# Fourier matmuls placed between the heads of a recurrence kernel's chunk loop, and small zero products in batch 0

## What is computed

```python
# B, H, S, D = 4, 8, 768, 48; DM = H * D = 384
scale = np.minimum(mag, 0.999) / (mag + 1e-06)          # mag = |a|
for t in range(S):                                       # complex decay per key dimension
    new_re = ar * S_re - ai * S_im
    new_im = ar * S_im + ai * S_re
    S_re, S_im = (new_re + kv, new_im)                   # kv = k_t outer v_t
    y[:, :, t] = np.einsum('bhd,bhde->bhe', q[:, :, t], S_re)
x = y as (B, S, DM)
u = x + real(fft(fft(x, axis=1), axis=2))                # Fourier mixing
u = u + relu(layernorm(u) @ w_ch1) @ w_ch2               # 384 -> 1536 -> 384
h = relu(u.T @ w_tok1) @ w_tok2, u = u + h.T             # second block: token mixing
out = u + relu(u @ w_ch1') @ w_ch2'
```

## Time and profile before

| What | Value |
|---|---|
| three timed runs | 1131.98, 1138.62, 1141.57 us; median 1138.62 |
| profiled execution | 1134.15 us, span 1132.4, mean TensorE clock 0.928 of full |
| busy share of the span | PE 89%, PEld 86%, DVE 48%, ACT 30% |
| edited phase | 0 to about 417 us |

### The profile page before, as it was taken

How to read it: one execution, slowest core, us unless ns; L and a number is a source line. 1 busy time by engine, 2 the same in 40 slices (tenths; PEclk the granted TensorE clock), 3 DMA queues, 4 the chain that set the end, 5 groups by cost and what they waited for, 6 DMA issues and landing times. The chain is left out here.

```text
span 1132.4 us, 15567 instructions
## 1 busy us (share of the span) xinstructions
PE 1008.8 (89%) x6082; PEld 971.8 (86%) x6082; DVE 538.2 (48%) x1040; ACT 341.4 (30%) x515; POOL 29.9 (3%) x15
## 2 busy tenths in 40 slices
PE   0469799989969973999999999968999999999998
PEld 0348699979969863999999999968999999999998
DVE  6798877897973338332432422225223322331411
ACT  6636545655621113121122112124121220310310
POOL 0000000000000004000000000004000000000000
PEclk9859759779969895999999999999999999999999
DMA  4559777765757013602102101001001000100000
GB/s 151 150 152 301 221 226 224 208 196 156 196 145 281 22 44 100 223 29 84 33 22 69 42 28 63 15 23 43 15 8 46 24 14 21 42 21 15 6 22 21
DMA packets 96887, 104.79 MB, mean 93 GB/s; under 512 B 13121, under 2 KB 90433, under 8 KB 96834
## 3 DMA queue, kind: packets, MB, share of 16 engines
q1 hardware_dynamic: 96834, 104.07, 29.7%
HBM read 70.93 MB, written 33.11 MB: 92 GB/s over the span
## 5 line engine op out<-in xcount | busy, mean ns | idle before, releaser
L1125 ACT ACTIVATE hh<-mbank 128x384 fp32r<-128x384 f32 x192 | 94.5, 492 | 370.8 <-PE mbank L1309 370.8
L1218 DVE SCALAR_TENSOR_TENSOR hl<-mbank,hh 128x384 fp32r<-128x384 f32 x192 | 107.1, 558 | 200.9 <-ACT hh L1125 200.9
L1307 PE MATMUL mbank<-nTh,w1h 128*128 128x384 f32 x576 | 193.9, 337 | 0.7 <-DVE w1l L1240 0.7
L1308 PE MATMUL mbank<-nTl,w1h 128*128 128x384 f32 x576 | 193.2, 335 | 0.0
L1309 PE MATMUL mbank<-nTh,w1l 128*128 128x384 f32 x576 | 193.2, 335 | 0.0
L1307 PE MATMUL mbank<-w2h,hh 128*128 128x384 f32 x576 | 193.1, 335 | 0.0
L1309 PE MATMUL mbank<-w2h,hl 128*128 128x384 f32 x576 | 192.4, 334 | 0.0
L1308 PE MATMUL mbank<-w2l,hh 128*128 128x384 f32 x576 | 192.4, 334 | 0.0
L1307 PEld LDWEIGHTS mbank<-nTh,w1h 128*128 128x128 f32 x576 | 108.8, 189 | 1.5 <-issue 1.3
L1308 PEld LDWEIGHTS mbank<-nTl,w1h 128*128 128x128 f32 x576 | 108.8, 189 | 0.0
L1309 PEld LDWEIGHTS mbank<-nTh,w1l 128*128 128x128 f32 x576 | 108.7, 189 | 0.0
(11 more groups left out here) (152 smaller groups left out, 1320.7 us busy)
## 6 DMA issues: line engine op xcount, KB each, us to landing
kT<-k_turn SPq DMA_DIRECT2D x24, 384.0 KB, 3.6
qT<-q_turn SPq DMA_DIRECT2D x24, 384.0 KB, 4.4
q_turn<-w_raw SPq DMA_DIRECT2D x30, 192.0 KB, 4.4
k_turn<-t SPq DMA_DIRECT2D x24, 192.0 KB, 4.0
k_turn<-w_early SPq DMA_DIRECT2D x24, 192.0 KB, 4.6
u_scratch<-y_sb SPq DMA_DIRECT2D x24, 192.0 KB, 3.1
w_raw<-in_moe_w_ch SPq DMA_DIRECT2D x2, 2304.0 KB, 10.3
x_early<-u_scratch SPq DMA_DIRECT2D x4, 1152.0 KB, 10.0
```

The costliest lines, as they stand in the source:

```text
L1125: nc.scalar.activation(hh[:, m, :], mm_bank[(g * (KF + TPG) + m) % 2][:, 0:TG], ACT.Relu).then_inc(h_high, 1)
L1218: nc.vector.scalar_tensor_tensor(out=hl[:, m, :], in0=mm_bank[(g * (KF + TPG) + m) % 2][:, 0:TG], scalar=0.0, in1=hh[:, m, :].bitcast(fp32 ...
L1307: nc.tensor.matmul(out, lh, rh, start=(n == 0), stop=False)
L1308: nc.tensor.matmul(out, lh, rl, start=False, stop=False)
```

## The change

TensorE's program alone is edited. (1) `sequence_transform` can issue single steps of its seven. (2) `fourier_beside(m, h)` runs behind head h's score and output: it issues that head's share of the block's 0, 7 or 14 steps, so one tile gives one step behind each of heads 1 to 7, and two tiles give one step behind heads 0 and 4 and two behind each of the others (the second tile begins behind head 4). (3) In batch 0 it issues one product of 193 zero columns for each head, and `keep_busy(3)` behind the update goes. (4) The wait for the wide tables moves ahead of `turn_keys(6)`. (5) A tile with number 0 or 1 waits for all of `a_ready`, the others as before, now ahead of their first step. The work at j = 1 and behind the loop keeps its order; `width_transform` is only written in two parts.

```diff
+            def sequence_transform(b, m, steps):
...
+                for n in steps:
+                    k_ = (n - 1) % KD
+                    if n == 0:
+                        if m < 2:
+                            pe.wait_ge(a_ready, (b + 1) * KD)
+                        else:
+                            pe.wait_ge(b_added, b * NT + m - 1)
+                        mm(out[:, 0:FH], alt[:, rows], a_mid[:, :], start=True, stop=False)
+                    elif n <= KD:
+                        mm(out[:, 0:FH], cs[:, k_, rows], a_sb[:, k_, 0:FH], start=False, stop=(k_ == KD - 1))
+                    else:
+                        last = mm(out[:, FH:2 * FH], ss[:, k_, rows], a_sb[:, k_, FH:2 * FH],
+                                  start=(k_ == 0), stop=(k_ == KD - 1))
+                    if n == SEQ - 1:
+                        last.then_inc(b_made, 1)
+
+            def fourier_beside(m, h):
+                b, j = m // NCH - 1, m % NCH
+                tiles = transformed_at(j)
+                if b < 0:
+                    mm(f_bank[0][:, 0:FH], ident[:, :], fold[:, 0, 0, 0:FH], start=True, stop=True)
+                for step in range(SEQ * len(tiles) * h // H, SEQ * len(tiles) * (h + 1) // H):
+                    if b >= 0:
+                        sequence_transform(b, tiles[step // SEQ], [step % SEQ])
...
+                if m == NCH:
+                    pe.wait_ge(wide_tables_in, 5 * 16)
                 if j < NCH - 1:
                     turn_keys(m)
...
                     score(m, h)
                     if m and h + ahead < H:
                         output(m - 1, h + ahead)
+                    fourier_beside(m, h)
...
-                if m < NCH:
-                    keep_busy(3)
-                if m == NCH:
-                    pe.wait_ge(wide_tables_in, 5 * 16)
...
-                if b:
-                    for n in transformed_at(j):
-                        sequence_transform(b - 1, n)
```

More of the change, by code:

```diff
@@ L706, in middle @@
                 last.then_inc(mid_made, 1)
-            def width_transform(b, m):
-                if m == 0:
-                    pe.wait_ge(folded, (b + 1) * KD)
-                    if b:
[L712 to L730, removed]
+            def width_transform(b, m, part):
+                if part == 0:
+                    if m == 0:
+                        pe.wait_ge(folded, (b + 1) * KD)
+                        if b:
+                            pe.wait_ge(b_added, b * NT)
+                    if m == 1:
+                        pe.wait_ge(mid_ready, b + 1)
+                    if m == 2:
+                        pe.wait_ge(a_ready, b * KD + 1)
+                for k_ in range(KD):
+                    last = mm(f_bank[(m + 1) % 2][:, part * FH:(part + 1) * FH],
+                              fold[:, part, k_, m * P:(m + 1) * P], (cd, sd)[part][:, k_, :],
+                              start=(k_ == 0), stop=(k_ == KD - 1))
+                if part == 1:
+                    last.then_inc(a_made, 1)
@@ L731, in sequence_transform @@
+            SEQ = 1 + 2 * KD
+            def sequence_transform(b, m, steps):
                 rows = slice(m * P, (m + 1) * P)
                 out = f_bank[m % 2]
[L733 to L738, removed]
@@ L739, in sequence_transform @@
-                last.then_inc(b_made, 1)
+                for n in steps:
[10 more added lines that the diff above has]
+                        last = mm(out[:, FH:2 * FH], ss[:, k_, rows], a_sb[:, k_, FH:2 * FH],
+                                  start=(k_ == 0), stop=(k_ == KD - 1))
+                    if n == SEQ - 1:
+                        last.then_inc(b_made, 1)
@@ L767, in _ @@
                     update(m)
-                if m < NCH:
-                    keep_busy(3)
-                if m == NCH:
-                    pe.wait_ge(wide_tables_in, 5 * 16)
                 if b and j == 1:
                     middle(b - 1)
-                    for n in range(KD):
-                        width_transform(b - 1, n)
-                if b:
-                    for n in transformed_at(j):
-                        sequence_transform(b - 1, n)
+                    for n, part in product(range(KD), range(2)):
+                        width_transform(b - 1, n, part)
                 if m:
@@ L788, in _ @@
             middle(B - 1)
-            for n in range(KD):
-                width_transform(B - 1, n)
+            for n, part in product(range(KD), range(2)):
+                width_transform(B - 1, n, part)
             for n in range(NT):
-                sequence_transform(B - 1, n)
+                sequence_transform(B - 1, n, range(SEQ))
 def token_by_token(nc, q, k, v, a_re, a_im, y_scratch):
```

## The result

The changed kernel's four runs have their median at 1174.54 us (1173.12 to 1190.13), the kernel before at 1138.86. The ratio is 1.0353, 95% interval [1.0269, 1.0436]: slower by 36 us between the medians (40 by the ratio), where the forecast of 1158 stood 19 above the three timed runs. The profiled execution took 1175.63 (span 1173.9), 41.4 more than that of before; the two phases behind the edited one are as long as they were.

A forecast was written before the change was run, and what follows sets the result against it. It took VectorE as the bound in blocks 14 to 19, TensorE in the last batch. Terms 8.6 + 10.4 + 0.5 + 1.0 = 20.5 us gave 1154.7 profiled, 1159 from the timed median; it took 1158, range 1142 to 1180.

The forecast's parts named there:

- late score: Blocks 8 and 14: steps ahead of the last score delay VectorE's masks, +2.2 us each.
- early adds: Tiles 3 and 5 in blocks 10, 11, 16, 17: TensorE waits for VectorE's adds, 1.5 and 3.3 us.
- The clock: Blocks 10, 11, 16, 17: TensorE's clock falls beside the new waits, 5.2 us per batch, +10.4 in all.
- Rival 3: Woven blocks: the clock falls and stays low through them, about +40 us, 1178; chance 0.12.
- What bounds it: Blocks 14 to 19: VectorE is the bound, working 66.31 of 68.90 us; last batch: TensorE, 54.69 of 56.
- Cover in block 15: Block 15: VectorE's 16.3 us before its masks hide TensorE's 12.4, +0; up to about 5 if cover goes.
- Batch 0: Batch 0: the wait for block 6's keys swallows a slip up to about 5 us; +0.5, bounds 0 to +8.
- rival 2: Start of batch 1: its low clock stretch goes too, some 12 us come back, 1136; chance 0.08.
- The 3.4 us that batch 1 was to get back: Batch 1: VectorE's waits of 1.64 and 1.75 us for late matmuls go if the clock holds, -3.4.
- Batch 3: Batch 3 and the end: order doesn't matter from block 20 on; +1.0 us, a clock fall up to 7.
- Blocks 20 to 23 keep their length: Blocks 20 to 23: sign that would show the forecast right, their length unchanged.

The follow-up runs named there:

- e5: The changed kernel plus two unread products of 384 columns ahead of the transposes of y in every block from 6 on: 1170.35 us.
- e6: The kernel before plus two unread products of 384 columns ahead of the transposes of y in every block from 6 on: 1148.62 us.
- e3: The kernel before with the Fourier steps woven singly between the update's matmuls, behind the last score: 1136.49 us.
- e4: The kernel before with the Fourier tiles in one dense piece ahead of the block's last score, behind head 6: 1159.45 us.
- e8: The kernel before with Fourier steps woven between the heads only in blocks j = 3 (two tiles): 1141.58 us.
- e2: The kernel before with only the change's batch 0 products and earlier wait for the wide tables, tiles in one piece behind the update: 1137.45 us.
- e7: The kernel before with Fourier steps woven between the heads only in batch 3 (blocks 18 to 23): 1140.98 us.
- g1: The kernel before plus ten products of 384 columns ahead of block 6's transposes and three behind its update, nothing woven: 1128.01 us.
- e1: The changed kernel with batch 0 as in the kernel before, so only the weave between the heads: 1175.18 us.
- e9: The kernel before with Fourier steps woven between the heads only in blocks j = 2 (8, 14, 20; one tile each): 1156.66 us.
- f1: The kernel before, nothing woven, with width transforms moved behind the scores of block j = 2 and tiles two each to j = 3, 4, 5: 1151.77 us.

## Why the prediction was wrong

The direction was right, and so were the late score and the early adds; the size was not. The term that failed is the clock's: the prediction charged it to blocks 10, 11, 16 and 17 alone and put nothing on blocks 8, 14 and 20. Rival 3 (1178) came nearest in its number, in part by luck. In blocks 10, 11, 16 and 17 it had 29.2 us in all, where the trace has 20.8; it put nothing on the clock in blocks 8 and 14, which took 5.8 us beyond the late score's 2.2 each, and had only "some" for batch 3's 11.8.

- **What bounds it, right but for a label.** The stretch read as blocks 14 to 19 (262.7 to 331.6) begins with block 14's masks, so it holds blocks 15 to 19; block 14 itself, with its 5.62 us of waiting, is bound by TensorE, as the terms have it.
- **Late score, right.** "+2.2" for a one-tile block is 2.4 to 2.8 at full clock (e5 against e6 and against before). e3 and e4 show that the side of the last score is what decides: the same steps cost nothing behind it, a dense piece ahead of it 21.5 us, late score and low clock together.
- **Early adds, right.** Forecast 3.3 us of waiting in block 17, measured 3.46. The forecast 1.5 showed as 1.2 in block 10 and not at all in block 16, where TensorE came to the tile later, at low clock.
- **Cover in block 15, right in the changed kernel,** and broken in e8 by a fall, at the price named.
- **Batch 0, right in its effect** (e2), because the wait for block 6's keys swallowed the slip. The slip itself was put too low: "about a microsecond" in rival 2, and block 5 ended 4.6 us later in the changed kernel (7.7 in e2).
- **The 3.4 us that batch 1 was to get back didn't come:** the clock fell in blocks 10 and 11 again. That the figure was right shows in e3, e6, e7, e8 and g1, whose traces have no fall there: block 11 takes 12.0 to 12.2 us in them, and 15.6 in the kernel before.
- **The clock, wrong.** The step that failed reads "I expect a fall in both": blocks 16 and 17 (and 10 and 11), 5.2 us for each of two batches, and no other block. In those blocks it was nearly the right size (16 and 17: 9.0 forecast, 11.8 measured). The changed kernel's trace has nine falls in blocks 9 to 23 besides those in the waits ahead of blocks 13 and 19, 82 us at low clock; the kernel before has one, of 13.7. Blocks 14 and 20 fell with no wait ahead of them. In every run whose block 14 or 20 was woven without filler the clock fell in it (7 of 7 blocks in the changed kernel, e1, e7 and e9), and in none of the 17 such blocks of the other orders, f1 and e5 aside. In all seven it fell 0.3 to 1.4 us after the start of the first woven step (271.50 and 271.8 in block 14), when one or two steps were out; the transposes, outputs and bare heads ahead of it are those of the kernel before. I had taken the fall to need a wait beside it, though the fall at 199 had none.
- **Batch 3, wrong in its size.** "I take +1.0 for both", with "up to 7" as the bound: 11.8 us in the profiled execution (6.6 in block 20, 5.2 in 21 to 23), about 4 between the medians for this batch alone (e7). "Blocks 20 to 23 keep their length", a sign that the prediction named, failed.

By the table, 12.4 of the 21 missing microseconds of the profiled execution (41.4 less the forecast's 20.5) are in blocks 8 (1.3), 14 (4.5) and 20 (6.6); the others are in 10 and 11 (3.4), 16 and 17 (2.8) and 21 to 23 (4.2), less 2.0 in batch 0. Low clock is shown as the cause in blocks 14 and 20 by e5, where filler took the fall away. For the rest it is argued from TensorE's 217.49 us at 0.76 against 187.90 at 0.89. What stays open is what a weave would cost with no fall at all, since e5 still had six falls, and why the clock falls when the first step stands beside a head and not when bare heads go on. That first step is a product over one partition (1x193), the other six are over 128; no run moved it by itself, so its share is not known.

The Trainium skill (TensorE: Matmul & The Clock Gate, section Why this matters for your kernels) speaks of idle gaps between bursts of matmuls; by it blocks 14 and 20 should have kept their clock. The runs don't agree: 7.30 of 7.60 us were busy ahead of block 14's fall, and 7.70 of 8.00 ahead of block 20's (366 to 374).

**Rival 2** priced the low stretch at the start of batch 1 at 12 us. g1 measured 10.1 in the blocks concerned, 8.2 in the medians (1136.25 against 1128.01). In the changed kernel the wait for the keys had shrunk from 7.24 to 2.75 us, and the clock fell there all the same, at 135.3.

## What to carry to other kernels

When two engines hand work to and fro, place filler work behind the last result that the other engine waits for, not ahead of it: a dense block that looks like dead time on its own engine can be the cover under which the other one works. Price every wait that moves with its instruction (here a bank's release) against the work that used to stand ahead of it. And products that nobody reads were worth their time in one place here, a wait of 7.2 us with short matmuls behind it (8.2 us gained); two in every block cost 11.8 us where 8 were expected. Elsewhere both have to be measured.

## Unexpected on the hardware

- The clock fell from 2.4 to 1.2 GHz in block 14 while TensorE was busy 7.30 of 7.60 us, and stayed low for 10.1 us of unbroken work (block 14 of the changed kernel).
- Filler of 1.3 us a block cost the kernel before 11.8 us, though TensorE was taken to be the bound in six blocks only (8 us of filler); its trace has a fall of 13.7 us in blocks 22 and 23 that the kernel before's does not have.
- Ten products in a wait of 7 us, and three behind the next update, kept the clock up for 40 us (1.00 against 0.70).
- In the kernel before, TensorE was busy for 28.57 of the 28.60 us behind that wait (136.6 to 165.2), and the clock stayed at 1.2 GHz throughout.
